# Alpha loaded later, the router weights' wait moved, GpSimd's w_in split held behind DVE's w2 parts, and the first token tile transposed from where it lands

## The reference

```python
attn_out = _attn_ref(q, k, v)            # (4, 8, 576, 64): softmax over earlier and own blocks of 64, times v
x = attn_out.transpose(0, 2, 1, 3).reshape(2304, 512)

# routed layer
do_compute = (x @ w_skip) > 0
e_idx = argmax(x @ w_gate)               # 8 experts
y = gate_w * (relu(x @ w1[e]) @ w2[e])   # 512 -> 1024 -> 512, own expert of each row
x = where(do_compute, x + y, x)

# dense layer
h = x @ w_in                             # 512 -> 2048
g = maximum(h, 0) + alpha * minimum(h, 0)
out = g @ w_out                          # 2048 -> 512
```

## Time and profile before

| | us |
|---|---|
| median of three runs | 886.57 |
| lowest and highest run | 886.46, 888.45 |
| profiled execution, its own time | 888.26 |
| its span in the profile | 886.4 |
| TensorE matmul busy | 822.2 (93%) |
| VectorE busy | 455.2 (51%) |
| ScalarE busy | 275.7 (31%) |
| GpSimd busy | 196.0 (22%) |

### The profile page before, as it was taken

How to read it: one execution, slowest core, us unless ns; L and a number is a source line. 1 busy time by engine, 2 the same in 40 slices (tenths; PEclk the granted TensorE clock), 3 DMA queues, 4 the chain that set the end, 5 groups by cost and what they waited for, 6 DMA issues and landing times.

```text
span 886.4 us, 15750 instructions
## 1 busy us (share of the span) xinstructions
PE 822.2 (93%) x5281; PEld 724.9 (82%) x5282; DVE 455.2 (51%) x917; ACT 275.7 (31%) x651; POOL 196.0 (22%) x191
## 2 busy tenths in 40 slices
PE   5799999999829799999949999999999999999997
PEld 5588888888629699999939889998998998998996
DVE  3477777777884632424644643444534444354432
ACT  5466656656433223113411112112112112112111
POOL 6224334332004314100248821001001001000000
PEclk9899999999959899999969999999999999999999
DMA  5386787563429665418733202002002002000001
GB/s 138 72 208 182 194 222 188 124 148 96 125 71 368 244 213 196 154 47 282 262 95 96 83 1 71 0 0 71 0 0 71 0 0 71 0 0 35 1 1 36
DMA packets 92951, 92.35 MB, mean 104 GB/s; under 512 B 64128, under 2 KB 65280, under 8 KB 92416
## 3 DMA queue, kind: packets, MB, share of 16 engines
q1 hardware_dynamic: 84352, 64.24, 25.3%
q0 software_dynamic: 4208, 14.95, 5.8%
q10 hardware_dynamic: 4368, 12.88, 4.0%
HBM read 64.78 MB, written 16.78 MB: 92 GB/s over the span
## 4 chain that ended last, share of the span: by engine, by line
PE 87%; DVE 3%; issue 3%; ACT 2%; DMA 2%; SPq 1%; POOL 0%; DVEq 0%; ACTq 0%; POOLq 0%
PE bank L905 23%; PE bank L916 22%; PE bank L855 10%; PE bank L869 8%; PE bank L740 5%; PE bank L751 4%; PE bank L728 3%; PE bank L704 2%; PE bank L774 2%; PE bank L722 2%; ACT p_sb L961 1%; PE bank L757 1%; PE bank L893 1%; PE bank L842 1%; DMA u_sb<-y_slots,from_i 1%
## 5 line engine op out<-in xcount | busy, mean ns | idle before, releaser
L1400 DVE TENSOR_SCALAR g_sb<-bank,alpha_sb 128x384 f32<-128x384 f32 x96 | 59.3, 618 | 218.4 <-PE bank L905 218.3
L1075 ACT CAST g_hi<-g_sb 128x384 fp32r<-128x384 f32 x96 | 49.4, 515 | 321.9 <-DVE g_sb L1402 321.9
L905 PE MATMUL bank<-u_hi,wi_hi 128*128 128x384 f32 x384 | 130.4, 339 | 1.4 <-DVE u_lo L1373 1.4
L905 PE MATMUL bank<-u_hi,wi_lo 128*128 128x384 f32 x384 | 130.4, 339 | 0.0
L905 PE MATMUL bank<-u_lo,wi_hi 128*128 128x384 f32 x384 | 129.8, 338 | 0.0
L916 PE MATMUL bank<-wo_lo,g_hi 128*128 128x512 f32 x288 | 113.8, 395 | 0.0
L916 PE MATMUL bank<-wo_hi,g_hi 128*128 128x512 f32 x288 | 112.9, 392 | 0.8 <-DVE g_lo L1406 0.8
L916 PE MATMUL bank<-wo_hi,g_lo 128*128 128x512 f32 x288 | 113.5, 394 | 0.0
L855 PEld LDWEIGHTS bank<-rows_t,w_sb 128*128 128x128 f32 x832 | 97.6, 197 | 3.0 <-DVE rows_t L1317 1.9
L855 PE MATMUL bank<-rows_t,w_sb 128*128 128x128 f32 x832 | 97.9, 280 | 1.5 <-DVE rows_t L1317 1.5
L961 ACT ACTIVATE p_sb<-bank,neg_max 128x128 f32<-128x128 f32 (+2 forms) x144 | 79.2, 552 | 54.2 <-DVE neg_max L1104 51.7
(11 more groups left out here) (170 smaller groups left out, 1252.1 us busy)
## 6 DMA issues: line engine op xcount, KB each, us to landing
w_sb<-in_moe_w_dram ACTq DMA_DIRECT2D x6, 2048.0 KB, 9.0
w_sb<-in_moe_w_dram SPq DMA_DIRECT2D x6, 2048.0 KB, 10.1
q_t<-q_t SPq DMA_DIRECT2D x64, 160.0 KB, 2.5
w_sb<-in_moe_w_dram SPq DMA_DIRECT2D x16, 512.0 KB, 4.9
v_nat<-in_v_dram SPq DMA_DIRECT2D x32, 128.0 KB, 2.4
y_out<-in_moe_w_out_dram POOLq DMA_DIRECT2D x16, 256.0 KB, 3.0
out_dram<-y_out SPq DMA_DIRECT2D x16, 256.0 KB, 2.7
qk_nat<-in_q_dram SPq DMA_DIRECT2D x30, 128.0 KB, 3.5
```

Source lines behind the costliest of these rows:

```text
L905: last = pe.matmul(dst, w[:, j, P * f:P * f + P], u[:, j, :], start=z == 0, stop=z == len(terms) - 1)
L1075: act.copy(g_hi[:, f % GB, :], g_sb[:, f % 2, :]).then_inc(g_hi_done, 1)
L1400: dve.tensor_scalar(g, a, 0.0, alpha_sb[:, f:f + 1], ALU.min, ALU.mult).then_inc(neg_done, 1)
```

## The change

It has three parts.

1. `alpha` moves. Its load goes from in front of SyncE's loop to behind the load of v for the last pair, on a semaphore of its own, and VectorE waits for it ahead of the last layer. TensorE's wait in front of the loop over pairs is gone; `to_rows` waits for the four remaining small loads (64 instead of 80).
2. The first tile of the routed layer is transposed from `rows_in`; ScalarE's copy of it is gone. All counts on `rows_copied` fall by one, and GpSimd's second gather waits for the transposes (`rows_tr`) rather than for the copy.
3. GpSimd waits for `second_split` to reach e+1, which is VectorE's second subtraction for expert e, ahead of both pieces of its w_in split (e is 1, then 3).

```diff
-            sp.dma_start(alpha_sb[:], alpha.rearrange("(t p) -> p t", p=P), allow_slow_non_contiguous=True).then_inc(small_loaded, 16)
             sp.wait_ge(zeros_set, 1)
...
             load_v(PAIRS - 1)
+            sp.dma_start(alpha_sb[:], alpha.rearrange("(t p) -> p t", p=P), allow_slow_non_contiguous=True).then_inc(alpha_loaded, 16)
...
                     pool.wait_ge(tokens_copied, g + 1)
-                    pool.wait_ge(rows_copied, g + 2)
+                    pool.wait_ge(rows_copied, g + 1)
...
             pick_rows(token_i[:, 0:1])
-            pool.wait_ge(rows_copied, 1)
+            pool.wait_ge(rows_tr, 1)
             pick_rows(token_i[:, 1:2])
...
                 if odd and t < LATE:
+                    pool.wait_ge(second_split, e + 1)
                     wi_rows(t)
...
             def to_rows(n):
 
+                pe.wait_ge(small_loaded, 64)
                 pe.wait_ge(o_evac, 2 * n + 2)
...
             pair(0, 0, first=True)
-            pe.wait_ge(small_loaded, 80)
...
             def rows_transposes(g):
-                pe.wait_ge(rows_copied, g + 1)
+                if isinstance(g, int):
+                    pe.wait_ge(rows_loaded, 16)
+                else:
+                    pe.wait_ge(rows_copied, g)
+                src = rows_in if isinstance(g, int) else rows
                 for j in range(KD):
-                    last = pe.transpose(RING[0][:, P * j:P * j + P], rows[:, P * j:P * j + P], ident[:])
+                    last = pe.transpose(RING[0][:, P * j:P * j + P], src[:, P * j:P * j + P], ident[:])
...
             def rows_copy(g):
                 act.wait_ge(rows_loaded, 16 * g + 16)
-                if not isinstance(g, int):
-                    act.wait_ge(rows_tr, g)
+                act.wait_ge(rows_tr, g)
                 act.copy(rows[:], rows_in[:]).then_inc(rows_copied, 1)
...
             act.wait_ge(routed, 1)
-            rows_copy(0)
...
+            dve.wait_ge(alpha_loaded, 16)
             first_row(0)
```

More of the change, by code:

```diff
@@ L232, in program @@
         small_loaded = sem("small_loaded")
+        alpha_loaded = sem("alpha_loaded")
         router_const = sem("router_const")
```

## The result

The changed kernel took **883.27 us** (median of nine, 878.53 to 883.86) against 888.18 us for the kernel before on the same chip: a ratio of 0.9941, 95% interval 0.9929 to 0.9954. It is 4.9 us faster where 12.35 were forecast, and it lies above the range of 871.5 to 877.6. Two more measurements of the same kernel later gave 0.993 and 0.992.

A forecast was written before the change was run, and what follows sets the result against it. TensorE, busy 822.2 of 886.4 us, bounds the kernel, so only its waits and slow-clock losses can pay. Savings of 6.63 (alpha) plus 5.72 (first tile and GpSimd's split), 12.35 us, take 886.57 to 874.2 us; range 871.5 to 877.6.

The forecast's parts named there:

- Part 1: Attention, pair 1: without alpha's wait TensorE saves 6.63 us, 4.57 of wait and 2.06 of slow matmuls.
- The rival in which alpha's wait is followed by another: Attention, pair 1: clock falls anyway or another wait comes; alpha's move gives 3 to 4.6 us, about 877; chance 0.07.
- Part 2: First routed tile: transposes start about 0.7 us sooner; second gather 0.5 us later at no cost; gain absorbed by a later wait.
- Part 3: Routed tile 1: GpSimd no longer collides with VectorE; 7.79 us alone, 5.72 together with the first tile's gain.
- That transfer does not come sooner: Expert 2's w2 load: DMA engines full at 424 GB/s, so rounding stays at 296.02, cutting the saving to 5.72 us.
- The clock: Rival at tile 2: clock falls in the new 1.8 to 2.5 us wait, costing 1.7 us, 875.9 us; chance 0.27.
- the transfer lands earlier: Rival at tile 2: expert 2's w2 arrives sooner or does not bind; saving 15.1 us, time 871.5; chance 0.09.
- the slower rival: Routed layer: GpSimd's new waits make it late to row gathers of tiles 4 and on; 892 us; chance 0.03.

The follow-up runs named there:

- e1: The kernel before with only alpha's load moved; 882.53 us, ratio 0.9937.
- e14: The changed kernel without its first-tile part, measured a second time; 877.35 us, ratio 0.9881.
- e15: The whole changed kernel with GpSimd's stage load issued ahead of the third row gather; 875.99 us, ratio 0.9868.
- e8: The changed kernel, unedited, measured again; 881.46 us, ratio 0.993.
- e11: The changed kernel without its first-tile part, first measurement; 877.83 us, ratio 0.9885.
- e7: The changed kernel with the next expert's w1 load issued on ScalarE behind the rounding of the w2 before it; 874.70 us, ratio 0.9854.
- e16: The changed kernel with the stage load ahead of the third gather and the zero fill behind tiles 0 and 1 and their w2 loads; 873.10 us, ratio 0.9833.
- e5: The changed kernel with the zero fill of unused row slots moved behind the last w2 load; 875.36 us, ratio 0.9855.
- e13: The changed kernel, unedited, measured a third time; 881.47 us, ratio 0.992.

## Why the prediction was wrong

**Part 1** was right in its mechanism and size: no wait, no new wait in pair 1, 6.71 us from the transposes on against a forecast of 6.63; by time it was 5.6 us in e1, within its bounds of 4.57 to 7.5. The rival in which alpha's wait is followed by another is out.

**Part 2** was right where it looked (the first w1 matmuls come 6.45 us behind the gather instead of 7.21, 0.76 saved against 0.7) and wrong in its price. The prediction said that the second gather would be 0.5 us later and that this was free, since tile 1's rows were needed 12 us later. The gather's delay was 0.54 us, and tile 1's rows were in time; but the step stopped at the rows and did not ask who stands behind the gather on GpSimd. There stood the stage load, 2.4 us later. With the part taken out (e14) 4.1 us come back, and with the stage load alone moved (e15) 5.5. That it is just these 2.4 us that cost is not shown: e15 sends the load out 7.8 us sooner than the change does, and e8 and e14 leave the same zero fill at different stage times.

**Part 3** was right about the collision of the two engines, about 4.48 us without it, and about what ends last next: the rounding behind a transfer, then 6.81 us to the w2 matmuls.

**The step that failed** is "That transfer does not come sooner": the sum let it land at its old distance, at 296.02 less part 1's 6.63, thus 289.39. Its issue moved by 7.13 us (282.33 to 275.20), a little more than that, but it took 18.34 us instead of 13.7, and the rounding came at 293.56, 4.17 us later than the sum had it. The evidence used was that the engines were full from 290 to 295 with 424 GB/s. That was true, and says nothing about which queue's bytes they moved. In the trace of before, w2 had 0.16 MB to go when w1 of expert 3 came in; in the change it had 1.00 MB.

**The clock** was a rival with a chance of 0.27 and a price of 1.7 us. It fell; the wait was longer than forecast (6.7 us instead of 1.8 to 2.5) and the matmuls took 8.41 us, 2.55 more than the 5.86 in the sum. The clock turned to 0.50 about 2.3 us after TensorE went idle, inside a gap of 4.38 us. e11 shows that no such gap is needed: its longest gap there is 1.89 us, up to 296.66, and the clock fell in it and the w2 matmuls took 7.17 us:

```profile
293.30:296.00 2.70, 0.69 (x5) 0.42 (x4) 2.70 (x2) 1.87 (x6) 1.14 (x1) 1.00 1.01 378
296.00:296.60 0.60, 0.00 (x0) 0.00 (x0) 0.60 (x3) 0.00 (x0) 0.60 (x1) 0.62 0.68 263
```

In e7 a gap of 1.88 us left the clock at 1.00. So waits of the forecast's length go either way. The Trainium skill's page "TensorE: Matmul & The Clock Gate", section "HAM oscillation — how this bites in real kernels", lets only a gap longer than these do that; e11 speaks against taking it strictly. Two numbers of this rival were off from the start. Its price began at 5.60 us, though the sum already held 5.86. And TensorE had not worked "only half the time" ahead of 25.81, it was busy for 4.90 of the 5.80 us before, which takes away one of its reasons for thinking the new wait safer.

The account: 12.35 forecast, less 4.17 (load) and 2.55 (clock) leaves 5.63, the lead seen at the tile behind. The old kernel lost 0.26 more at a later tile (5.86 instead of 5.60) and the change 1.2 at the dense layer, which makes 4.7, the difference of the spans.

With the load freed (e16) the kernel takes 873.1 us against 888.76 for the kernel before on its chip. The ratio of 0.9833 is 14.8 us, more than the 12.35 of the forecast and near the 15.1 of the rival "the transfer lands earlier"; that 873.1 stands so near to 874.2 is in part luck of the base. The opportunity was there, and the change as written does not collect it. One sum of the slower rival does not come out: with two pieces, each over by the delay less 17 us, the kernel is slower from a delay of some 23 us, not 31; nothing hung on it.

## What to carry to other kernels

When an edit frees a stage, take the next transfer in line and write down, queue by queue, the bytes ahead of it in its own queue and the loads that will run beside it; "the engines are full" sets a total, not a share. A step that moves an instruction on an in-order queue must be followed to the last thing issued behind it, prefetches above all. Bulk work with a late deadline (here the zero fill) belongs behind the urgent loads, though not so far back that it meets the start of the next stage (3 us in e5), and if runs of one kernel fall into two groups, look for two transfers whose order is a close race.

## What the runs showed of the hardware

- In the change, two queues that loaded at the same time got the same number of packets (338 and 337), not the same bytes: 1.38 MB and 0.69 MB in 5 us. At the end of a load this need not hold (397 and 26 packets in 4 us before).
- The same 2 MB load took 9.9 us (e5) to 19.9 us (e13) from issue to use, by what stood before and beside it.
- A row gather issued 0.5 us later, 1.20 us instead of 0.68 behind the first zero-fill transfer, kept GpSimd waiting for 5.57 us instead of 3.70.
- The granted clock fell about 2.3 us after TensorE went idle, although it had been busy without a gap in the 30 us before. With a longest gap of 1.89 us it fell in e11; with one of 1.88 us it held in e7.
